# A fused attention and two-MLP kernel: weights, conversions and last row blocks in another order

## The reference

```python
q_d, k_d, v_d = (t.reshape(B, H, S // 4, 4, D).mean(axis=3) for t in (q, k, v))
out_up = np.repeat(sm_attn(q_d, k_d, v_d), 4, axis=2)          # softmax attention on averages of 4
scores = np.where(abs(pos[:, None] - pos[None, :]) < 4, scale * q @ k.T, -1e9)
out_local = softmax(scores) @ v                                 # a band of 7 keys
x = (out_up + out_local) as [2304 tokens, 512]

h = x @ w_in;  g = h - np.tanh(h);  x = g @ w_out               # w_in 512x2048, w_out 2048x512
gate = 1 / (1 + np.exp(-(x @ w_gate)));  val = x @ w_val        # both 512x1536
return (gate * val) @ w_out2                                    # 1536x512
```

## Time and profile before

| | us |
|---|---|
| median of 3 runs | 909.3 |
| the profiled execution's own time | 911.66 |
| its span, first to last instruction | 909.9 |
| PE busy | 884.9 (97%) |
| PE weight loads busy | 832.6 (92%) |
| DVE busy | 580.4 (64%) |
| ACT busy | 380.8 (42%) |
| POOL busy | 289.5 (32%) |
| mean granted TensorE clock | 0.996 of full |

### The profile page before, as it was taken

The page is one execution under the profiler, slowest core; times in us unless marked ns, Lnnn a source line. Parts: engine busy times, 40 slices in busy tenths (PEclk is TensorE's granted clock), DMA queues, the critical chain, the costliest instruction groups (busy, mean ns, idle before and its releaser), DMA issues.

```text
span 909.9 us, 15664 instructions
## 1 busy us (share of the span) xinstructions
PE 884.9 (97%) x6088; PEld 832.6 (92%) x6088; DVE 580.4 (64%) x921; ACT 380.8 (42%) x720; POOL 289.5 (32%) x237
## 2 busy tenths in 40 slices
PE   7998999998999999999998999999999999999997
PEld 5877899998999999999998899999999999999996
DVE  8999876667766668565676556576444466444445
ACT  4777854435333344233344444443222243222221
POOL 5899775672030001020047657612200001000000
PEclk9999999999999999999999999999999999999999
DMA  8875597669454636454225777779755555755511
GB/s 258 247 224 163 179 374 266 230 239 359 173 209 158 220 140 223 152 201 181 95 68 202 284 278 278 277 292 356 277 209 208 209 208 208 262 224 208 208 47 69
DMA packets 36137, 197.01 MB, mean 217 GB/s; under 512 B 3712, under 2 KB 5248, under 8 KB 23008
## 3 DMA queue, kind: packets, MB, share of 16 engines
q1 hardware_dynamic: 29584, 162.16, 48.2%
q0 software_dynamic: 4032, 29.36, 8.5%
q10 hardware_dynamic: 2448, 4.49, 1.6%
HBM read 139.90 MB, written 56.10 MB: 215 GB/s over the span
## 4 chain that ended last, share of the span: by engine, by line
PE 84%; POOL 7%; DVE 3%; issue 3%; DMA 2%; ACT 2%; SPq 0%; ACTq 0%; DVEq 0%; POOLq 0%
PE banks L843 45%; PE banks L915 18%; PE banks L1031 16%; DMA mid_raw<-in_moe_w_out_dram 1%; PE banks L817 1%; POOL win L616 1%; POOL prob L584 1%; PE banks L789 1%; PE banks L774 1%; POOL v_four L577 1%; PE banks L834 1%; PE banks L806 1%; PE banks L763 1%; POOL mid L630 1%; POOL win L624 0%
## 5 line engine op out<-in xcount | busy, mean ns | idle before, releaser
L843 PE MATMUL banks<-x_op,pair 128*128 128x384 f32 x1512 | 278.5, 336 | 1.7 <-DVE cg_sum L1579 1.7
L843 PEld LDWEIGHTS banks<-x_op,pair 128*128 128x128 f32 x1512 | 266.7, 189 | 9.7 <-DVE cg_sum L1579 2.1
L915 PE MATMUL banks<-g_parts,mid 128*128 128x384 f32 x1152 | 226.9, 335 | 4.3 <-DVE x_all L1484 4.1
L915 PEld LDWEIGHTS banks<-g_parts,mid 128*128 128x128 f32 x1152 | 202.5, 188 | 5.9 <-DVE x_all L1484 5.9
L843 PE MATMUL banks<-x_op,win 128*128 128x384 f32 x1008 | 202.4, 336 | 3.1 <-ACT c_sum L1147 3.0
L843 PEld LDWEIGHTS banks<-x_op,win 128*128 128x128 f32 x1008 | 177.6, 189 | 4.1 <-ACT c_sum L1147 3.4
L1031 PE MATMUL banks<-wout,p_parts 128*128 128x512 f32 x648 | 163.6, 393 | 1.7 <-issue 1.7
L1484 DVE TENSOR_TENSOR x_all<-banks,x_all 128x384 f32<-128x384 f32 x168 | 92.6, 555 | 83.5 <-PE banks L915 83.1
L1031 PEld LDWEIGHTS banks<-wout,p_parts 128*128 128x128 f32 x648 | 120.2, 188 | 22.6 <-issue 2.1
L1604 DVE TENSOR_TENSOR x_all<-banks,x_all 128x512 f32<-128x512 f32 x90 | 62.1, 690 | 113.7 <-PE banks L1031 113.7
L643 POOL DMA_DIRECT2D wout<-kept_out x12 | 6.5, 540 | 211.4 <-PE banks L1031 211.4
(11 more groups left out here) (98 smaller groups left out, 984.4 us busy)
## 6 DMA issues: line engine op xcount, KB each, us to landing
pair<-kept_pair SPq DMA_DIRECT2D x24, 1792.0 KB, 10.3
win<-kept_in SPq DMA_DIRECT2D x16, 1792.0 KB, 7.3
kept_pair<-pair SPq DMA_DIRECT2D x12, 1792.0 KB, 11.8
mid<-kept_mid POOLq DMA_DIRECT2D x16, 1024.0 KB, 5.1
kept_in<-win SPq DMA_DIRECT2D x8, 1792.0 KB, 6.8
wout<-kept_out POOLq DMA_DIRECT2D x12, 1024.0 KB, 11.6
kept_mid<-mid SPq DMA_DIRECT2D x8, 1024.0 KB, 5.0
kept_out<-wout SPq DMA_DIRECT2D x6, 1024.0 KB, 14.0
```

The source lines that it names most:

```text
L843: mm = pe.matmul(bk[:, 0:T], weights[:, w, p - 1, kk, :], x_op[:, p - 1, x, kk, :], start=(first and kk == 0 and a == 0), stop=(last and k ...
L915: mm = pe.matmul(bk[:, 0:T], w[:, wp, f, m * P:(m + 1) * P], g[:, gp, 2 * f + t, :], start=(f == 0 and a == 0), stop=(f == 1 and a == 2))
```

## The change

It changes no arithmetic; the order of instructions, the amount in one of them (val 0's low part is made in two halves) and the waits that go with this.

1. SP: in the loop over quads the raw mid load stands ahead of the load of a kept win. This differs from before in one iteration, n = 6: mid 7's raw weights ahead of unit 8's kept win.
2. End of the first MLP: gate 0's raw weights are loaded one quad earlier, POOL makes their sums in quad 22's iteration and the low part in the last one, ahead of val 0's sums and `x_last_sum`. ACT makes gate 0's high part in the middle of the last quad, and those of gate 1 and val 1 ahead of the second MLP's first copies instead of within round 0.
3. DVE: the split x_low(NS, 2) leaves the last quad for the blocks behind it, val 0's low part is cut in two halves between blocks, and val 1's is made ahead of round 0 instead of within it. The semaphore `s_vlo` counts one more (`val_lows(c)` = c + 2).
4. Last round, m = 17: row blocks 2 and 3 of round 16 stand behind the last products, and DVE adds them behind the last gated values.

The parts below come in this order: SP's `load_raw2` and loop, POOL, PE's last round, ACT (`first_quad`, the border, the rounds), DVE (the border, the rounds).

```diff
-                        sp.wait_ge(s_p1, 7 * (N1 - 1))
+                        sp.wait_ge(s_p1, 7 * (N1 - 2 + a))
...
                 if 4 <= n + 2 < Q1:
                     load_raw(n + 2)
-                elif Q1 <= n + 2 < N1:
+                if n + 1 < Q1:
+                    load_raw_mid(n + 1)
+                if Q1 <= n + 2 < N1:
                     load_win(n + 2)
                 if n + 1 < Q1:
-                    load_raw_mid(n + 1)
                     keep_win(n + 1)
...
+                if n == N1 - 2:
+                    weight_sums(Q1)
                 if n == N1 - 1:
-                    weight_sums(Q1)
+                    weight_low(Q1)
+                    weight_sums(Q1 + 1)
                 if n % Q1 == Q1 - 1:
                     x_last_sum(n // Q1 + 1)
-                if n == N1 - 1:
-                    weight_sums(Q1 + 1)
-                    weight_low(Q1)
...
                 second_product(m, 5)
-                row_block(m - 1, 2)
+                if m < N2 - 1:
+                    row_block(m - 1, 2)
                 second_product(m, 4)
-                row_block(m - 1, 3)
+                if m < N2 - 1:
+                    row_block(m - 1, 3)
                 second_product(m, 3)
+                if m == N2 - 1:
+                    row_block(m - 1, 2)
+                    row_block(m - 1, 3)
...
                     x_high(s, 6)
                 if 3 <= n + 1 < Q1:
                     weight_high(n + 1)
+                if n == N1 - 1:
+                    weight_high(Q1)
...
                 if n == N1 - 1:
                     g_high(n, 1)
-                    weight_high(Q1)
...
             x_high(NS, 3)
+            weight_high(Q1 + 2)
+            weight_high(Q1 + 3)
...
-                if m + 1 < Q2:
+                if 1 <= m and m + 1 < Q2:
                     weight_high(Q1 + 2 * m + 2)
...
+            def val_low(c, part):
...
             add_block(N1 - 2, 4)
             g_low(N1 - 1, 1)
-            for i in range(5, BLOCKS):
-                add_block(N1 - 2, i)
+            add_block(N1 - 2, 5)
+            add_block(N1 - 2, 6)
+            x_low(NS, 2)
+            add_block(N1 - 2, 7)
             add_block(N1 - 1, 0)
+            x_low(NS, 5)
             add_block(N1 - 1, 1)
-            x_low(NS, 5)
             add_block(N1 - 1, 2)
+            val_low(0, slice(0, WS // 2))
             add_block(N1 - 1, 3)
-            val_low(0)
-            for i in range(4, BLOCKS):
-                add_block(N1 - 1, i)
+            add_block(N1 - 1, 4)
+            val_low(0, slice(WS // 2, WS))
+            add_block(N1 - 1, 5)
+            add_block(N1 - 1, 6)
+            add_block(N1 - 1, 7)
             x_low(NS, 4)
             x_low(NS, 3)
+            val_low(1, slice(0, WS))
...
-                add_rows(m - 1, 3)
-                if m + 1 < Q2:
-                    val_low(m + 1)
+                if m < N2 - 1:
+                    add_rows(m - 1, 3)
+                if 1 <= m and m + 1 < Q2:
+                    val_low(m + 1, slice(0, WS))
```

More of the change, by code:

```diff
@@ L326, in lows, with val_lows @@
             return 4 if su == 0 else su + 3
+        def val_lows(c):
+            return c + 2
         def splits(s, p):
@@ L485, in keep_pair @@
                 sp.dma_start(kept_pair[0][c], flat_f32(pair[c % 2][0][:, :, :, :, :])).then_inc(s_kept2[c % 2], 16)
-                sp.wait_ge(s_vlo, c + 1)
+                sp.wait_ge(s_vlo, val_lows(c))
                 sp.dma_start(kept_pair[1][c], flat_f32(pair[c % 2][1][:, :, :, :, :])).then_inc(s_kept2[c % 2], 16)
@@ L988, in second_product @@
                         if m < Q2:
-                            pe.wait_ge(*((s_wlo, lows(Q1 + m)), (s_vlo, m + 1))[v_])
+                            pe.wait_ge(*((s_wlo, lows(Q1 + m)), (s_vlo, val_lows(m)))[v_])
                         mm = product(a, w, p, True, False)
@@ L1524, in first_quad @@
                 add_block(n - 1, 3)
-                if last:
+                if last and n < N1 - 1:
                     x_low(s, 2)
@@ L1540, in _ @@
                 first_quad(n)
+            def val_low(c, part):
+                dst, raw = pair[c % 2][1], pair_raw[c % 2][1]
+                dve.wait_ge(s_whi, highs(Q1 + 2 * c + 1))
+                dve.tensor_tensor(dst[:, 1, :, :, :].rearrange("p o k n -> p (o k n)")[:, part], raw[:, :, :].rearrange("p o n -> p (o n)")[:, part],
+                                  dst[:, 0, :, :, :].rearrange("p o k n -> p (o k n)")[:, part].bitcast(F32), ALU.subtract).then_inc(s_vlo, 1)
             add_block(N1 - 2, 4)
             g_low(N1 - 1, 1)
-            for i in range(5, BLOCKS):
-                add_block(N1 - 2, i)
-            def val_low(c):
-                dst, raw = pair[c % 2][1], pair_raw[c % 2][1]
-                dve.wait_ge(s_whi, highs(Q1 + 2 * c + 1))
-                dve.tensor_tensor(dst[:, 1, :, :, :].rearrange("p o k n -> p (o k n)"), raw[:, :, :].rearrange("p o n -> p (o n)"),
-                                  dst[:, 0, :, :, :].rearrange("p o k n -> p (o k n)").bitcast(F32), ALU.subtract).then_inc(s_vlo, 1)
+            add_block(N1 - 2, 5)
+            add_block(N1 - 2, 6)
+            x_low(NS, 2)
+            add_block(N1 - 2, 7)
             add_block(N1 - 1, 0)
+            x_low(NS, 5)
             add_block(N1 - 1, 1)
-            x_low(NS, 5)
             add_block(N1 - 1, 2)
+            val_low(0, slice(0, WS // 2))
             add_block(N1 - 1, 3)
-            val_low(0)
-            for i in range(4, BLOCKS):
-                add_block(N1 - 1, i)
+            add_block(N1 - 1, 4)
[3 more added lines that the diff above has]
+            add_block(N1 - 1, 7)
             x_low(NS, 4)
             x_low(NS, 3)
+            val_low(1, slice(0, WS))
             def add_c2(m, i, v_):
@@ L1627, in _ @@
                     x_low(s, 2)
-                add_rows(m - 1, 2)
+                if m < N2 - 1:
+                    add_rows(m - 1, 2)
                 gated(m, C22)
@@ L1635, in _ @@
                 gated(m, C21)
-                add_rows(m - 1, 3)
-                if m + 1 < Q2:
-                    val_low(m + 1)
+                if m < N2 - 1:
+                    add_rows(m - 1, 3)
+                if 1 <= m and m + 1 < Q2:
+                    val_low(m + 1, slice(0, WS))
                 gated(m, C12)
-                add_rows(m - 1, 4)
-                add_rows(m - 1, 5)
+                if m < N2 - 1:
+                    add_rows(m - 1, 4)
+                    add_rows(m - 1, 5)
+            add_rows(N2 - 2, 2)
             p_low(N2 - 1, 1)
+            for tb in range(3, TB):
+                add_rows(N2 - 2, tb)
             for tb in range(TB):
```

## The result

The changed kernel takes 898.88 us in the median of four runs (898.0 to 899.88), the one before 909.84 in four (907.8 to 911.5). The ratio is 0.9874, 95% interval [0.9853, 0.9895]: 11.5 us faster, between 9.6 and 13.4. Timed again on another occasion it is 898.22 against 909.52, ratio 0.9873 [0.9851, 0.9896]. The profiled execution took 898.21 us with a span of 896.4, which is 13.5 less than the 909.9 of the one before. The forecast was 896.0 in a range of 893.2 to 902.5, from a sum of 13.4; both medians lie in the range, but just above the 894 to 898 to which it gave 0.70. Two things need an explanation: why the profile moved as forecast, and why the times moved 2 us less.

A forecast was written before the change was run, and what follows sets the result against it. PE was taken as the bound, so only its idle or half-clock time could be won. 5.27 + 2.7 + 3.7 + 1.69 = 13.4 us off the median 909.3 gave 895.9, rounded 896.0; range 893.2 to 902.5.

The forecast's parts named there:

- A: First MLP, mid 7 loaded ahead of the kept win: PE's stall for ACT's copy and half clock go, 5.27 us.
- B: Border between the MLPs: reordered DVE and POOL work cuts PE's waits for DVE's adds, 2.7 of 5.38 us.
- new stall of 1.0: First block behind the last quad: PE waits 1.0 us because DVE's adds come later, at 471.7.
- the lock: Border: DVE and POOL exclude each other from a shared port for a whole instruction, leaving 2.65 us of stalls.
- sharing: Border, the alternative: DVE and POOL share bandwidth, and nearly all of 5.4 us is gained.
- C: Round 0 of the second MLP: the 1.75 us wait for DVE's gated value and the half clock go, 3.7 us.
- D: End of the last round: PE's gap ahead of the last six row blocks goes, 1.69 us, bounds 1.0 and 1.69.
- the late transfer: Rival: mid 7 lands at 204 or later anyway; A brings 0 to 2, total 899 to 901 us; chance 0.10.
- the slower side: Rival: val 1's sums on POOL delay ACT's first copy, PE stops 10.7 us in round 0; slower; chance 0.03.
- DVE's eating of B: Rival: DVE's new stalls eat all of B, quad 23's late start costs two more; 901 us; chance 0.07.
- The list on ACT: Rival: conversions ahead of ACT's first copies stop PE 1 to 3 us in round 0; 899.5 us; chance 0.10.

The follow-up runs named there:

- second profile of before: The kernel before, unchanged, profiled once more: time 909.34 us, span 907.5 us.
- part A alone: The kernel before with only mid 7's raw weights loaded ahead of unit 8's kept win: ratio 0.9964, 3.3 us faster.
- part D alone: The kernel before with only row blocks 2 and 3 of round 16 behind the last products, DVE's adds to match: ratio 0.9977, 2.1 us faster.
- C alone: The kernel before with only gate 1's and val 1's conversions ahead of ACT's first copies and val 1's low part ahead of round 0: ratio 0.9974, 2.4 us faster.

## Why the prediction was right, and where it was off

- **A, 5.27.** The mechanism held at each step: mid 7 landed at 199.2 (199 to 201 forecast), the win at 205.4 (205), PE did not wait. Between the two profiles it is 4.89 (268.39 - 263.50) and not 5.27: the 0.38 are lost in the changed kernel too, at the first block of the quad, which starts 0.27 late and takes 0.11 longer than the others. The term was 3.05 for the stall and 2.2 for the clock, and I said that no stall means no half clock. There it held, but the stall didn't mean half clock either: three profiles of the same kernel have it once. The term is 2.8 to 3.0 us, and some 1.9 more only in such executions.
- **B, 2.7.** Measured 2.82 (19.94 to 17.12). No run has B alone; its share is read from the border in the traces. The second MLP starts 18.16 us after the last quad's last product begins (18.0 to 18.6 forecast), but PE's listed waits for DVE's adds sum to 1.3 where the forecast's sign was 2 to 3, the rest of the 2.56 being in waits too short for the list. The new stall of 1.0 is 0.98, x_low 1.51 (466.64 to 468.2 forecast, 1.56), the halves of val_low 1.38 and 1.20. This is the term that the lock decides; with sharing it would have been 5.4, and the run without POOL's long instruction shows the lock.
- **C, 3.7.** The wait of 1.75 went, and the first copy had 0.95 us to spare, 0.6 forecast. Between the two profiles it is 3.74, but 1.5 of it is the half clock again: in the second profile of before round 0 to the first row block is 23.03 (505.37 + 5.48 - 0.16 - 487.66), so the term is 2.2.
- **D, 1.69.** The gap went as forecast, but the last round is 2.05 us shorter, more than the 1.69 that was also the bound: the stop cost PE 1.8 by the distance of its pieces, and row blocks in a row take 1.36 each where those between products took 1.39.
- **The sum.** 13.4 against 13.5 in the profiles: 4.89 + 2.82 + 3.74 + 2.05. That it fits to 0.1 is in part luck, since A was 0.4 too large and D 0.4 too small, and since the profile of the changed kernel had no half clock at all, as six of its ten timed executions. Without half clock the terms are 2.9 + 2.8 + 2.2 + 2.05 = 9.95, and the executions at full clock are 9.9 apart. The times moved 10.96 to 11.5; the rest is the clock, 1.7 us between the medians of all executions. Part of the stretches has nothing to do with the four places: the one in the attention stands in five of the eight profiles of kernels that have at least one of the places, and in one of the five without. Behind 100 us there are six in those eight profiles and none in those five, in both cases counts too small for a rate.

The step that failed is the last one: "This execution was 2.4 us over the median 909.3, and I take the difference, not the ratio". The 2.4 us were no offset to subtract on both sides. They came from the two stretches at half clock that this execution had, at a cost of some 3.5 us where a typical one loses 2.15, and the sum had counted them in full as gain. The sign of it stood in the runs: the profiled execution was slower than all three. The right working is 9.9 for the stalls and 1.7 for the clock, of which the first follows from the rows once the half clock is taken out of them, and the second only from more executions.

Of the rivals, the late transfer, the slower side and DVE's eating of B did not come. The list on ACT exists, with 0.15 us where C stands alone.

## What to carry to other kernels

A profile is one draw. Where TensorE's clock falls behind a stall, count the stall as certain and the half clock as a chance, compare executions with the same mean clock, and look where the profiled execution lies among the timed ones before you carry its sum to the median. On an in-order engine a late transfer is paid by what is queued behind the instruction that waits for it, so a small urgent load belongs ahead of a large one with slack; and long GpSimd instructions belong where VectorE has no work with two inputs in SBUF.

## What the runs showed of the hardware

- The same kernel with the same idle stretches of PE (2.5 to 3.05, 2.12, 1.75 us) had the clock at 0.5 at 209 and 506 in one execution and only at 13 in two others. Also a run with waits of at most 2.12 us behind the first quad (part A alone) had it, at 481 to 484. Which one it is I could not tell from these traces, and what decides it no run here shows.
- Half clock costs only what no wait covers: behind A's stall 1.9 to 2.1 us, in round 0 1.5 to 1.6, at the border 0.65 (part A alone) and 0.8 (part D alone), for stretches of the same length.
- The lock works in both directions, and the waiting time counts as busy in the rows: DVE's val 1 took 4.85 us for 2.0 of work in the run of C alone, and POOL's weight_low 4.78 for 4.06 in the changed kernel, where it started behind DVE. A busy share of VectorE or GpSimd is then no measure of work.

```profile
490.21 4.85 DVE L1552 TENSOR_TENSOR pair<-pair_raw,pair 128x1792 fp32r<-128x1792 f32 x1 [0.96 <-ACT pair L1103]
```

```profile
488.40 4.77 POOL L616 TENSOR_TENSOR pair<-pair_raw,pair 128x1792 fp32r<-128x1792 f32 x1
```

Here POOL gets the port at about 489.1, after DVE's x_low, and has it to 493.17; DVE's val_low, issued at 490.21, ends 1.89 later, at 495.06.
